# An even batch's leftover tokens held for the odd batch's tile, and the first batch's convolution and value products in other slots

## The chip, the cores and the metric

The kernel runs on one NeuronCore of one Trainium2 chip. The metric is device time in microseconds, the median over executions of the whole program. Before the change it is 1050.89 us, median of 3 runs (1049.84 to 1052.85). All arithmetic is in fp32; products marked fp32r use a high and a low part of each operand.

## What is computed

For 4 batches of 576 tokens, three blocks run one behind the other. The first is attention with 8 heads of 64 that keeps only the 32 largest scores of each row; the second a gated block with a causal convolution over tokens; the third a Fourier mixing with a normalisation and a two-layer network:

```python
scores = scale * np.matmul(q, k.transpose(0, 1, 3, 2))
kth = np.partition(scores, -top_k, axis=-1)[..., -top_k:-top_k + 1]      # top_k = 32
attn = softmax(np.where(scores >= kth, scores, -1e9));  x = attn @ v     # x: (4, 576, 512)

gate_pre += conv_w[k] * xp[:, k:k + S, :]                                # 5 taps
x = (1 / (1 + exp(-gate_pre)) * (x @ w_val)) @ w_out

mixed = np.real(np.fft.fft(np.fft.fft(x, axis=1), axis=2))
u = x + mixed
un = (u - mean(u)) / sqrt(var(u) + 1e-6)
out = u + np.maximum(un @ w_ch1, 0) @ w_ch2                              # 512 -> 2048 -> 512
```

## The kernel before

**Slots.** The whole program is one list of slots, and each engine walks through it in its own instruction stream. Slot s starts the scores of attention tile s. There are 16 pairs of heads with 9 tiles each, so 36 tiles a batch and 144 in all. The stages of one tile lie behind each other by slots: VectorE's search for the 32 largest (`search`, L1007: four MAX8 and three MATCH_REPLACE8 per tile) one and two slots later, the exponential on ScalarE four later, the transposes of the probabilities on TensorE five later (L588), and the product with v (`attend`, L591) six later.

**The two later blocks of a batch** are a list of steps (`STEPS`, L109), spread by `steps_by_slot` (L160) over the 36 slots that follow a batch's attention, so batch 0's steps lie in slots 42 to 77, beside batch 1's attention. Each step has an estimated cost (`COST`, L117), and the planner fills the slots evenly by it. The steps are: `val` (8 value products), `zed` and `seq` (the Fourier mixing), `proj` (5 projections), `trn` (5 transposes of normalised tokens), `ch0` and `ch1` (the hidden layers over 16 chunks, for two groups of tiles). Batch 3 has no attention beside it; its steps have one slot each at the end.

**Row tiles.** 576 tokens are four tiles of 128 and 64 leftover tokens (`ROWS`, L47; `LEFT` is 64). Tile number 4 (`NR - 1`) is the leftover one. For an even batch its tokens lie in partitions 0 to 63, for an odd one in 64 to 127 (`half_of`, L74). Before the change both batches of a pair do `proj` 4, the normalisation and `trn` 4 on 64 tokens each, with results side by side in `un_hi`, `un_lo` and `u[4]`; the hidden layers over the leftover tokens are already run once for the pair, in the odd batch's `ch1` (`GROUPS`, L58).

**Around the projection.** `project` (L710) multiplies the gated values with w_out, 16 matmuls a tile. `sequence` (L693) makes the mixing sums, ScalarE copies them to `ab`, and GpSimd's `plus_minus` (L1225) makes `pm` of them. VectorE's `make_u` (L1071) adds both into `u[r]` and takes the statistics (bn_stats, bn_aggr), GpSimd's `deviation` (L1238) makes 1/sqrt of the variance, VectorE's `normalise` (L1088) writes `un`, TensorE transposes it (`transpose_un`, L729), ScalarE stores it twice (L923, L924) and GpSimd subtracts (L1257).

**First batch.** Its convolution is on TensorE with diagonal matrices (`convolve`, L625, placed by `CONV0_AT`, L145), its tanh reads the result from PSUM (`TANH0_AT`). Two value products of batch 0 are begun early, at slot 39 (`VAL0_AT`, L156, `early_values`, L652): 6 products, each of two instructions. For batches 1 to 3 the convolution is on VectorE: one instruction for each tap of a range of tokens (`CONV_AT`, L150; `conv`, L1055). Only the last pair's is cut into two ranges, FRONT (tokens 0 to 383) and BACK (384 to 575).

**Order within a slot** on TensorE (L796 to L814): scores, transposes, the first step, `attend`, the convolution, early values, the other steps. At slot 42 alone (`CONV_LAST`) the convolution stands ahead of the first step. On VectorE (L1138 to L1154): half of the search, the first step, the other half, the convolution, the other steps. Each engine works in order, so an instruction that waits holds all behind it.

**Start.** SyncE's queue issues two loads of k for head 0 and four of q and k for head 1 (L517 to L519), ScalarE's queue two of q for head 0 (L937). The low parts of the first keys are made on VectorE, those of the first queries of head 0 on GpSimd (`low_queries`, L1158).

## Time and profile before

| | us |
|---|---|
| median of 3 runs | 1050.89 |
| lowest, highest | 1049.84, 1052.85 |
| the profiled execution | 1052.33 |
| its span, first to last instruction | 1050.6 |

The profile is of one execution. Its engines are TensorE (PE; PEld is its weight loads), VectorE (DVE), ScalarE (ACT), GpSimd (POOL) and SyncE (SP), whose stream only issues transfers. Busy time of PE is the union of instructions whose ends are modelled, so a PE that is nearly always busy need not be at its peak rate.

Attention's search ends near 857 us of the span; from there only batch 3's steps run. The steps of batch 0 start near 211 us, those of batch 1 near 427 us, of batch 2 near 666 us.

### The profile page before, as it was taken

The page shows a single profiled execution, that of the slowest core. Times are in us where ns is not written, and L with a number is a line of the kernel's source. Part 1 is how long each engine was busy: PE and PEld are TensorE (multiplying, and loading weights), DVE is VectorE, ACT ScalarE, POOL GpSimd, SP SyncE. Part 2 cuts the span into 40 slices and gives each one's busy share as a digit, 9 for nine tenths or more (in the row PEclk, how much of TensorE's full clock was granted, in tenths as well). Part 3 has the DMA queues.
Part 4 walks back from the last instruction along what each step waited for, and adds up shares of the span by engine and source line. Part 5 has one row for each costly group of instructions (what it writes and reads, how often), then busy time and mean ns, then how long its engine had stood idle before and what let it go on. Part 6 is the DMA issues. An engine that isn't in the chain of part 4 may idle for free.

```text
span 1050.6 us, 20124 instructions
## 1 busy us (share of the span) xinstructions
PE 972.2 (93%) x6784; PEld 831.6 (79%) x6784; DVE 839.0 (80%) x1824; ACT 647.2 (62%) x1421; POOL 408.2 (39%) x544
## 2 busy tenths in 40 slices
PE   4876767899999999999999999999999999999997
PEld 3555655678888898878898889878888888888896
DVE  7999999988999999989999977898999973120000
ACT  5887687856777767665777666666676762122121
POOL 2675544534533333244333332243442222543221
PEclk9997688799999999999999999999999999999999
DMA  9565656560186778511777655510676776059873
GB/s 237 181 202 167 220 185 200 173 215 24 26 293 228 284 265 293 177 35 34 274 269 259 200 202 198 163 35 24 214 262 244 261 252 231 1 199 358 297 248 129
DMA packets 84549, 203.80 MB, mean 194 GB/s; under 512 B 9056, under 2 KB 30304, under 8 KB 84448
## 3 DMA queue, kind: packets, MB, share of 16 engines
q1 hardware_dynamic: 84288, 202.22, 57.2%
q8 instruction: 55, 0.90, 0.4%
q10 hardware_dynamic: 160, 0.30, 0.1%
q14 instruction: 46, 0.38, 0.1%
HBM read 178.89 MB, written 23.59 MB: 193 GB/s over the span
## 4 chain that ended last, share of the span: by engine, by line
PE 77%; DVE 8%; issue 6%; ACT 6%; POOL 1%; DMA 0%; SPq 0%; ACTq 0%; DVEq 0%; POOLq 0%
PE p_m L757 18%; PE p_m L774 18%; PE p_t L604 9%; PE p_t L588 7%; PE p_s L574 7%; PE p_m L725 5%; PE p_m L647 4%; DVE rest L1004 3%; DVE top L993 3%; PE p_m L615 3%; PE p_m L706 3%; PE p_m L635 2%; PE p_t L608 2%; ACT prob L852 1%; ACT pT L866 1%
## 5 line engine op out<-in xcount | busy, mean ns | idle before, releaser
L993 DVE MAX8 top<-rest 128x8 f32<-128x576 f32 x432 | 310.3, 746 | 0.1
L1266 POOL TENSOR_TENSOR hid_lo<-hid,hid_hi 128x256 fp32r<-128x256 f32 (+1 forms) x128 | 107.5, 840 | 298.2 <-ACT hid_hi L934 298.2
L1004 DVE MATCH_REPLACE8 rest<-top,rest 128x576 f32<-128x576 f32 x288 | 214.1, 744 | 0.0
L774 PE MATMUL p_m<-w_st,hid_hi 128*128 128x512 f32 x576 | 181.3, 396 | 1.6 <-ACT hid_hi L934 0.7
L757 PE MATMUL p_m<-un_hi,w_st 128*128 128x256 f32 (+1 forms) x1024 | 164.2, 303 | 0.0
L840 ACT ACTIVATE s_sb<-p_s 128x576 f32<-128x576 f32 x144 | 93.1, 647 | 105.5 <-PE p_s L574 105.3
L757 PEld LDWEIGHTS p_m<-un_hi,w_st 128*128 128x128 f32 x1024 | 143.5, 188 | 5.6 <-issue 1.9
L588 PE MATMUL p_t<-id_sb,prob 128*128 128x128 f32 x720 | 111.6, 288 | 27.6 <-ACT prob L858 27.2
L933 ACT ACTIVATE hid<-p_m 128x256 f32<-128x256 f32 (+1 forms) x128 | 51.8, 405 | 128.5 <-PE p_m L757 127.6
L604 PE MATMUL p_t<-pT,v_sb 128*64 128x128 f32 (+1 forms) x1600 | 108.6, 288 | 22.9 <-ACT pT L866 22.9
L604 PEld LDWEIGHTS p_t<-pT,v_sb 128*64 128x64 f32 x1600 | 89.0, 149 | 48.6 <-ACT pT L866 29.6
L574 PE MATMUL p_s<-k_hi,q_st 128*128 128x288 f32 x320 | 108.9, 355 | 14.9 <-POOL q_st L1164 8.8
L858 ACT ACTIVATE prob<-prob,bias 128x576 f32<-128x576 f32 x144 | 111.8, 776 | 16.8 <-ACT prob L852 0.8
L588 PEld LDWEIGHTS p_t<-id_sb,prob 128*128 128x128 f32 x720 | 90.1, 148 | 35.4 <-ACT prob L858 33.9
L774 PEld LDWEIGHTS p_m<-w_st,hid_hi 128*128 128x128 f32 x576 | 101.1, 188 | 18.6 <-POOL hid_lo L1266 2.9
L774 PE MATMUL p_m<-w_st,hid_lo 128*128 128x512 f32 x288 | 113.6, 394 | 0.0
L993 DVE MAX8 top<-s_sb 128x8 f32<-128x576 f32 x144 | 108.8, 755 | 3.7 <-ACT s_sb L840 3.6
L852 ACT ACTIVATE prob<-s_sb,top 128x576 f32<-128x576 f32 x144 | 110.9, 770 | 0.0
L1004 DVE MATCH_REPLACE8 rest<-top,s_sb 128x576 f32<-128x576 f32 x144 | 107.1, 744 | 0.0
L866 ACT ACTIVATE pT<-p_t 128x640 f32<-128x640 f32 x144 | 101.3, 704 | 8.6 <-PE p_t L588 8.4
L1100 DVE TENSOR_TENSOR u<-p_m,u 128x512 f32<-128x512 f32 x18 | 11.5, 684 | 111.3 <-PE p_m L774 111.3
L574 PE MATMUL p_s<-k_lo,q_st 128*128 128x288 f32 x320 | 94.5, 310 | 0.0
(117 smaller groups left out, 1650.3 us busy)
## 6 DMA issues: line engine op xcount, KB each, us to landing
w_st<-w_split SPq DMA_DIRECT2D x256, 512.0 KB, 4.6
w_split<-w_st SPq DMA_DIRECT2D x32, 512.0 KB, 3.3
k_raw<-kT SPq DMA_DIRECT2D x62, 144.0 KB, 3.0
q_raw<-qT SPq DMA_DIRECT2D x60, 144.0 KB, 2.9
u<-w_ch SPq DMA_DIRECT2D x32, 256.0 KB, 3.9
v_sb<-v SPq DMA_DIRECT2D x16, 256.0 KB, 3.1
w_st<-wout_split SPq DMA_DIRECT2D x16, 256.0 KB, 3.9
out<-u SPq DMA_DIRECT2D x16, 256.0 KB, 2.4
```

The lines of the kernel that those rows point to most:

```text
L574: mm = pe.matmul(p_s[:, o, 0:HALF_S], q_st[h][p % 2][:, cols], k[:, o * HALF_S:o * HALF_S + HALF_S], start=n == 0, stop=n == len(parts) - 1)
L588: mm = pe.transpose(p_t[:, c * P:c * P + P], prob[t % 3][:, c * P:c * P + P], id_sb[:, :])
L604: pe.matmul(p_o[D * h:D * h + D, 0, 0:n], v_sb[p % 2][:, c, D * h:D * h + D], pT[tt % 3][:, c, c0:c0 + n], start=c == 0, stop=c == NCH - 1 ...
L757: mm = pe.matmul(mbank(hidden_bank(b, g, f), n), w1_st[i % NB1][:, w, k, :], x[:, k, at:at + n], start=part + k == 0, stop=part + k == KC + 1)
L774: mm = pe.matmul(mbank(j), h[i % 2][:, P * j:P * j + P], w2_st[i % NB2][:, w, :], start=f == 0 and part == 0, stop=f == FC - 1 and part == 2)
L840: act.activation(s_sb[t % NS][:, :].rearrange("p (o n) -> p o n", o=2), p_s[:, :, 0:HALF_S], ACT.Copy, scale=SCALE).then_inc(s_copy, 1)
L852: act.activation(prob[t % 3][:, 0:S], s_sb[t % NS][:, :], ACT.Prelu, bias=kth, scale=-1.0, alpha=1.0 / BIG).then_inc(s_drop, 1)
L858: act.activation(prob[t % 3][:, 0:S], prob[t % 3][:, 0:S], ACT.Exp, bias=bias[t % NK][:, :], scale=-BIG, accum_out=psum_row[:, t % NK:t % ...
L866: act.activation(pT[t % 3][:, :, :].rearrange("p c n -> p (c n)"), p_t[:, 0:SP], ACT.Copy).then_inc(s_pT, 1)
L993: found = dve.max(top[t % NK][:, 8 * n:8 * n + 8], (rest[t % 2] if n else s_sb[t % NS])[:, :])
L1004: chained(dve.match_replace(rest[t % 2][:, :], top[t % NK][:, 8 * n:8 * n + 8], (rest[t % 2] if n else s_sb[t % NS])[:, :], LOWEST), t)
L1266: pool.tensor_tensor(hid_lo[i % 2][:, 0:width(b, g)], hid[:, 0:width(b, g)], hid_hi[i % 2][:, 0:width(b, g)].bitcast(F32), ALU.subtract).t ...
```

## The change

An even batch leaves out `proj` 4 and `trn` 4. Its gated leftover values wait in `gv_hi` and `gv_lo`, its mixing sums for these tokens are written by GpSimd straight into `u[4]`, partitions 0 to 63. The odd batch's `proj` 4 then works on 128 tokens, one VectorE instruction adds the even half, and statistics, normalisation, transposes and the stores behind them run once on 128 tokens. The semaphore counts follow (`us`, `outs`). The planner spreads an even batch's remaining 56 steps anew.

Several other things are in the same change. The hidden layer of an even batch alternates between two PSUM banks from chunk 10 on, instead of 12 (`TRANSPOSED`). For batch 0 the convolution of the last pair's first half goes from slot 41 to 39, the second half stays at slot 42 but stands behind the first step, and the early value products go from slot 39 to slots 35 and 37, three products at each. The last tanh of batch 0 stands later in ScalarE's slot. For batches 1 to 3 the last pair's convolution is cut into three ranges: FRONT (384 tokens) at slots 39 and 40, NEXT (128) at 41 and BACK (64) at 42, instead of FRONT at 39 to 41 and BACK (192) at 42 (slots counted from the batch's start). At the start ScalarE's queue issues head 1's two loads of k, and VectorE makes the first low queries instead of GpSimd.

```diff
-CONV0_AT = {14: (0, 0), 16: (0, 1), 23: (1, 0), 25: (1, 1), 32: (2, 0), 34: (2, 1), 41: (3, 0), 42: (3, 1)}
-CONV_LAST = max(CONV0_AT)
+CONV0_AT = {14: (0, 0), 16: (0, 1), 23: (1, 0), 25: (1, 1), 32: (2, 0), 34: (2, 1), 39: (3, 0), 42: (3, 1)}
-WHOLE, FRONT, BACK = (0, S), (0, 3 * P), (3 * P, S)
+WHOLE, FRONT, NEXT, BACK = (0, S), (0, 3 * P), (3 * P, 4 * P), (4 * P, S)
-           39: [(3, FRONT, (0, 1))], 40: [(3, FRONT, (2, 3))], 41: [(3, FRONT, (4,))], 42: [(3, BACK, range(TAPS))]}
-CONVS = TAPS * (KC + 1)
-VAL0_AT, VAL0 = 39, 2
+           39: [(3, FRONT, (0, 1, 2))], 40: [(3, FRONT, (3, 4))], 41: [(3, NEXT, range(TAPS))], 42: [(3, BACK, range(TAPS))]}
+CONVS = TAPS * (KC + 2)
+VAL0_AT = {35: 0, 37: 1}
...
+LAST_TILE = [("proj", NR - 1), ("trn", NR - 1)]
-        steps = [(what, b, n) for what, n in STEPS]
+        steps = [(what, b, n) for what, n in STEPS if b % 2 or (what, n) not in LAST_TILE]
...
+TRANSPOSED = [10, 12]
-        return 3 if f == 1 or f >= 12 and f % 2 == 0 else 2
+        return 3 if f == 1 or f >= TRANSPOSED[b % 2] and f % 2 == 0 else 2
...
-                load_qk(0, 1)
+                for half in range(2):
+                    sp.dma_start(raw(0, 1)[0][D * half:D * half + D, :], qT[0, 1]).then_inc(s_qk_in[1], 16)
...
-                    bank = mbank(PROJ_BANK[r])[out_rows(b, r), :]
+                    bank = mbank(PROJ_BANK[r])
...
-                    if s == CONV_LAST:
-                        convolve(*CONV0_AT[s])
                     for x in plan[s][0:1]:
                         step(*x)
                     if unit_due(s):
                         attend(s - ATTEND)
-                    if s in CONV0_AT and s != CONV_LAST:
+                    if s in CONV0_AT:
                         convolve(*CONV0_AT[s])
-                    if s == VAL0_AT:
-                        early_values()
+                    if s in VAL0_AT:
+                        early_values(VAL0_AT[s])
...
+                for half in range(2):
+                    act.dma_start(raw(0, 1)[1][D * half:D * half + D, :], kT[0, 1]).then_inc(s_qk_in[1], 16)
                 high_keys(0, 0)
...
-                    if s in TANH0_AT:
+                    if TANH0_AT.get(s, KC - 1) < KC - 1:
                         gate_tanh(0, TANH0_AT[s])
...
+                    if TANH0_AT.get(s) == KC - 1:
+                        gate_tanh(0, KC - 1)
...
+                    at, made = slice(0, P), us(b) + 2 * (r + 1)
+                    if r == NR - 1:
+                        at, made = rows(b, r), us(b + 1)
+                        early = rows(b - 1, r)
+                        dve.tensor_tensor(u[r][early, :], y[early, :], u[r][early, :], ALU.add).then_inc(m_u, 1)
+                    ur = u[r][at, :]
                     dve.tensor_tensor(ur[:, 0:NCOS], y[at, 0:NCOS], pm[at, lo, :], ALU.add).then_inc(m_u, 1)
                     dve.tensor_tensor(ur[:, NCOS:DM], y[at, NCOS:DM], pm[at, hi, NCOS - 2:0:-1], ALU.add).then_inc(m_u, 1)
-                    dve.wait_ge(m_u, 2 * (NR * b + r + 1))
-                    dve.bn_stats(stats[at, r, :], ur).then_inc(m_st, 1)
+                    dve.wait_ge(m_u, made)
+                    dve.bn_stats(stats[:, r, :], u[r][:, :]).then_inc(m_st, 1)
...
+                dve.wait_ge(s_hi, 2)
+                dve.tensor_tensor(q_st[0][0][0:D, 0:S], q_raw[0:D, :], q_st[0][0][0:D, 0:S].bitcast(F32),
                                   ALU.subtract).then_inc(s_lo[0], 1)
                 low_queries(0)
...
+                    a, bb = ab[at, 1:NCOS - 1], ab[at, NCOS:DM]
+                    if g == 2 and b % 2 == 0:
+                        if b:
+                            pool.wait_ge(m_put, 16 * puts(b))
+                        to = u[NR - 1][at, :]
+                        pool.tensor_tensor(to[:, 1:NCOS - 1], a, bb, ALU.subtract).then_inc(m_pm, 1)
+                        pool.tensor_tensor(to[:, DM - 1:NCOS - 1:-1], a, bb, ALU.add).then_inc(m_pm, 1)
+                        for n in (0, NCOS - 1):
+                            pool.tensor_copy(to[:, n:n + 1], ab[at, n:n + 1]).then_inc(m_pm, 1)
+                        return
...
                 pool.wait_ge(s_zero, FILLS)
-                low_queries(0, 0)
```

## Rows read from the trace of the kernel before

**Rows 1.** The page, part 1: busy us, share of the span, instructions.
```profile
PE 972.2 (93%) x6784; PEld 831.6 (79%) x6784; DVE 839.0 (80%) x1824; ACT 647.2 (62%) x1421; POOL 408.2 (39%) x544
```

**Rows 2.** Windows: stretch, its us, each engine's busy us, PE clock, DMA share, GB/s.
```profile
0.00:198.00 198.00, 139.90 (x874) 109.38 (x875) 190.32 (x409) 147.44 (x301) 101.45 (x133) 0.83 0.64 197
198.00:208.80 10.80, 9.20 (x85) 7.58 (x84) 9.79 (x21) 9.62 (x22) 7.68 (x10) 0.98 0.47 165
208.80:272.00 63.20, 62.10 (x421) 51.94 (x420) 54.70 (x129) 39.82 (x86) 25.37 (x38) 1.00 0.31 106
272.00:453.00 181.00, 176.35 (x1395) 153.56 (x1393) 179.73 (x390) 128.03 (x292) 65.40 (x85) 1.00 0.67 232
453.00:473.00 20.00, 19.86 (x116) 17.14 (x117) 15.56 (x35) 14.45 (x30) 11.03 (x14) 0.91 0.00 1
497.00:608.00 111.00, 109.97 (x849) 98.40 (x849) 107.17 (x224) 77.56 (x177) 41.59 (x52) 1.00 0.73 246
664.00:693.00 29.00, 27.04 (x195) 21.79 (x191) 28.79 (x69) 17.96 (x39) 8.30 (x12) 1.00 0.40 122
728.00:861.00 133.00, 130.75 (x1048) 114.89 (x1047) 130.06 (x279) 96.49 (x222) 44.63 (x61) 1.00 0.68 232
```

**Rows 3.** The chain that ended last, start: start us, length us, what.
```profile
4.18 4.23 DMA x_new<-kT
```

**Rows 4.** The page, part 6: issues, KB each, median us to landing.
```profile
k_raw<-kT SPq DMA_DIRECT2D x62, 144.0 KB, 3.0
```

**Rows 5.** Timeline at the start: start, us, engine, line, operation, [idle before, releaser].
```profile
8.54 0.61 PE L574 MATMUL p_s<-k_hi,q_st 128*128 128x288 f32 x1 [8.54 <-POOL q_st L1164]
9.98 0.74 DVE L1038 TENSOR_TENSOR k_lo<-x_new,k_hi 128x576 fp32r<-128x576 f32 x1
```

**Rows 6.** Timeline, slots 39 to 43.
```profile
198.28 3.15 PE L647 MATMUL p_m<-x_new,wslot 128*128 128x257 f32 x12
...
207.89 2.69 PE L635 MATMUL p_m<-x_new,u 128*128 128x288 f32 x10
...
208.85 0.17 DVE L1051 TENSOR_SCALAR rinv<-psum_row 128x2 f32<-128x2 f32 x1 [0.98 <-ACT prob L858]
...
211.49 2.59 PE L635 MATMUL p_m<-x_new,u 128*128 128x288 f32 x10
...
214.56 0.42 DVE L1113 SCALAR_TENSOR_TENSOR gv<-gate,p_m 128x257 f32<-128x257 f32 x1 [2.56 <-PE p_m L647]
...
216.66 0.77 PE L588 MATMUL p_t<-id_sb,prob 128*128 128x128 f32 x5 [1.07 <-ACT prob L858]
```

**Rows 7.** The chain that ended last, batch 0's projection of tile 4.
```profile
280.58 2.80 PE p_m L725 x16
```

**Rows 8.** Timeline: tile 4 of batch 0 on DVE; a 64-token transpose on PE.
```profile
285.93 0.41 DVE L1081 TENSOR_TENSOR u<-p_m,pm 64x257 f32<-64x257 f32 x1
...
287.52 1.38 DVE L993 MAX8 top<-rest 128x8 f32<-128x576 f32 x2
...
321.94 0.53 DVE L1094 TENSOR_SCALAR un<-u,mv,rstd 64x512 f32<-64x512 f32 x1
322.39 1.41 DVE L993 MAX8 top<-rest 128x8 f32<-128x576 f32 x2
...
957.15 0.46 PE L742 MATMUL p_m<-id_sb,un 64*128 64x64 f32 x4
```

**Rows 9.** Groups by line and shape: operation, shape, count, busy us, mean ns, idle.
```profile
L1067 DVE SCALAR_TENSOR_TENSOR gate<-x_new,cw_sb,gate 128x384 f32<-128x384 f32 x12 | 9.2, 766 | 0.2
...
L1067 DVE SCALAR_TENSOR_TENSOR gate<-x_new,cw_sb,gate 128x192 f32<-128x192 f32 x12 | 5.0, 419 | 0.4
...
L1113 DVE SCALAR_TENSOR_TENSOR gv<-gate,p_m 128x63 f32<-128x63 f32 x16 | 3.4, 213 | 6.0 <-PE p_m L647 6.0
```

**Rows 10.** Timeline at the start of batch 1's and batch 2's steps.
```profile
453.14 0.65 PE L682 MATMUL p_m<-wfeat,gv 128*64 128x257 f32 x4 [2.57 <-DVE gv L1113]
...
693.40 1.12 PE L682 MATMUL p_m<-wfeat,gv 128*64 128x257 f32 x4 [2.36 <-DVE gv L1113]
```

More of the change, by code:

```diff
@@ L394, in folded, with tile_cols @@
             return gate[:, c, o * HALF + P * m:o * HALF + P * m + P]
[L396 to L401 removed]
+        def tile_cols(r):
+            return slice(ROWS[r][0], ROWS[r][0] + P)
         def w_out_half(b, k, h):
@@ L650, in value_products, with early_values @@
                     return mm
-                def early_values():
+                def early_values(j):
                     pe.wait_ge(m_wval, 16)
                     pe.wait_ge(s_feat_ev, KC)
-                    for j in range(VAL0):
-                        value_products(0, j, range(KC - 1))
+                    value_products(0, j, range(KC - 1))
                 def values(b, j):
@@ L672, in values @@
                         pe.wait_ge(m_tanh, KC)
-                    value_products(b, j, range(KC - 1 if b == 0 and j < VAL0 else 0, KC)).then_inc(m_val, 1)
+                    value_products(b, j, range(KC - 1 if b == 0 and j in VAL0_AT.values() else 0, KC)).then_inc(m_val, 1)
                 def zed(b, m):
@@ L724, in project @@
                             for c0, c1, w in w_out_half(b, k, h):
-                                mm = pe.matmul(bank[:, c0:c1], x[:, k, gv_cols(b, r)], w, start=n + k == 0,
+                                mm = pe.matmul(bank[:, c0:c1], x[:, k, tile_cols(r)], w, start=n + k == 0,
                                                stop=n == 2 and k == KC - 1, skip_group_check=True)
@@ L751, in hidden @@
                         pe.wait_ge(m_hev, hidden_before(i) + 1)
-                    if g == 0 and f == 12:
-                        pe.wait_ge(m_unT, 2 * NR * (b + 1))
+                    if g == 0 and f == TRANSPOSED[b % 2]:
+                        pe.wait_ge(m_unT, 2 * outs(b + 1))
                     at, n = HALF * g, width(b, g)
@@ L1057, in conv @@
                     n0, n1 = part
-                    dve.wait_ge(s_x, 5 * p + (3 if part == FRONT else 5))
+                    dve.wait_ge(s_x, 5 * p + {FRONT: 3, NEXT: 4}.get(part, 5))
                     if c == 0:
@@ L1072, in make_u @@
                     g = [0, 0, 1, 1, 2][r]
-                    at = rows(b, r)
                     lo, hi = (1, 0) if r in (1, 3) else (0, 1)
@@ L1117, in step @@
                         finish(b, int(what == "ch1"))
-                    if (what, n) in NORM_AT:
+                    if (what, n) in NORM_AT and outs(b) + NORM_AT[what, n] < outs(b + 1):
                         normalise(b, NORM_AT[what, n])
```

79 lines of the change are left out of this document (35 added, 44 removed).

## The prediction

> **What bounds the kernel now.** The first view is the busy shares of the page. TensorE reads 93% and VectorE 80% [rows 1], and taken over the whole span this would make the case one of TensorE's work alone. It does not hold stage by stage, so the second view is the busy time by windows [rows 2]. The reader is to look there for the engine whose busy time equals the length of the stretch.
>
> Up to 198 us it is VectorE. The table shows 190.3 of 198 us busy, and the missing part is the start, before the first scores. TensorE has 139.9 and its clock is granted at 0.83 of full, a mixture of 1.2 and 2.4 GHz. From 208.8 to 272 us it is TensorE: 62.1 of 63.2, while VectorE stands idle for 8.5 us. From 272 to 453 us both columns are nearly full, and here the two have to be told apart: VectorE lacks 1.3 us of 181, TensorE 4.7 us. So VectorE sets the end of that stretch and TensorE follows with some slack. The same holds from 728 to 861 us (VectorE lacks 2.9, most of it at the very end where its search is over, TensorE 2.3) and from 664 to 693 us (0.2 against 2.0). In 497 to 608 us neither has more than 4 us.
>
> The Trainium skill, Perfetto Trace Analysis, section Identifying the Most-Contended Engine, says that busy matmul time is no good measure for TensorE and that the busy share of weight loads should be read instead, with plain occupancy for VectorE. In this case's trace that is 79% against VectorE's 80% [rows 1], which goes with two engines that take turns. By the other reading, TensorE everywhere, the sum would be that of the first rival below.
>
> The third view is the timeline at the places where one engine waits for the other, used below.
>
> **The start.** ScalarE's queue takes over two of head 1's four loads. Today the last of the four is issued at 4.18 us and lands 4.23 us later [rows 3], against a median of 3.0 us for such loads [rows 4], so it stands in line behind the others and an earlier issue shortens little. The four issues on SyncE are 0.64 us apart, so two fewer ahead of the last one can give at most 1.3 us, and at worst nothing. I take 0.2, near the row that shows the line. VectorE also takes over the low queries that TensorE's first scores wait for [rows 5]. It costs one operation of about 0.75 us, and there VectorE is idle and waits for head 1's data. Its last operation before the search begins, at 9.98 us [rows 5], depends on that data and not on the first scores. Cover gone, it would cost 0.75 us. **Sum: 0.2 gained.**
>
> The Trainium skill, Trainium Kernel Development and Optimization, section Key Constraints, says that queues of several engines interleave on the same 16 DMA engines and save only the issue time. By it the gain is at most the 1.3 us of issue. The row of 4.23 us says less.
>
> **Slots 35 to 43, batch 0.** Today slot 39 holds 12 instructions of early value products, 3.15 us [rows 6]. In their place comes half a convolution, 10 instructions, 2.69 us [rows 6]. So slot 39 does not get longer as long as the clock is the same. The value products go to slots 35 and 37, where TensorE waits for the exponentials: it is idle for 58 of the 198 us before [rows 2], which is 1.5 us a slot over 39 slots. Half of them last 1.6 us at full clock, about 3 at half. What these two slots can't hide is some tenths, and the scores that follow have slack because VectorE is behind. I cost them at nothing; with no cover it would be 3 us.
>
> Slot 41 loses its convolution, 2.69 us, so scores 42 come that much earlier. In slot 42 the other half, 2.59 us, no longer stands ahead of the first value product, for which VectorE waits 2.56 us today [rows 6]. TensorE's wait of 1.07 us for an exponential [rows 6] goes too, because ScalarE's last tanh, which waits for the convolution, now stands behind that exponential. From slot 43 on TensorE is the bound, so it counts: 2.69 and 1.07 are 3.8 at most. VectorE's idle time up to there, 0.98 and 2.56 [rows 6], is 3.5, and it can't come further forward than that without becoming the late one. **I take 3.3, with 0.5 and 3.8 as ends.** What is late next is TensorE's own list of value products.
>
> **The leftover tile in an even batch.** On TensorE there go 16 matmuls, 2.80 us [rows 7], and 4 transposes, 0.46 [rows 8], together 3.3 us. On VectorE the tile occupies 285.93 to 287.52, which is 1.59 us, and its normalisation 321.94 to 322.39, 0.45 us [rows 8]: together 2.04 us. Both lie in a stretch where VectorE is the late engine, so 2.04 counts and TensorE's other 1.3 us become idle time. ScalarE and GpSimd lose work too; their busy shares of 62 and 39% [rows 1] leave that without effect. **Twice 2.0 is 4.1 us gained**, with 3.3 each as the upper end.
>
> In the odd batch nothing is saved. VectorE has one more addition, over 512 columns; by the 257-column one of 0.41 us [rows 8] it takes some 0.7. In batch 1 it lies ahead of the stretch from 497 us, where VectorE has under 4 us of room [rows 2], so between 0 and 0.7, and I take the middle: **0.35 lost**. In batch 3 it lies beside GpSimd's work and costs nothing. The transposes take 128 columns for 64, and weight loads as well: **0.15 lost** in the tail, where TensorE is alone. GpSimd's `plus_minus` in an even batch has as many instructions as before. For batch 2 it waits for the stores of batch 1, issued some ten slots earlier; behind it in GpSimd's stream stand low parts of the next keys, and nobody waits for them at once. SyncE's two waits for the last projection come one projection sooner, and the weight loads and query loads behind them too. The bank alternation from chunk 10 takes away waits on TensorE in a stretch where it has slack: nothing.
>
> **Narrow convolution, batches 1 to 3.** On VectorE five taps of 192 columns (0.42 us each [rows 9], 2.1 together) become five of 128 and five of 64. A 63-column instruction of the same kind takes 0.21 [rows 9] and between the two I get 0.33 for 128, so the ten take 2.7 us: 0.6 more. The ends are 0.3, by the slope from 384 to 192 columns (766 to 419 ns), and 2.1, if a narrow one costs as much as one of 192. In batch 1 it stands in VectorE's stretch: **0.6 lost**. For batch 2 the extra lies ahead of 664 us, where TensorE is the bound, and what remains behind is five taps of 64 for five of 192, 1.0 us less. There TensorE waits 2.36 us for the gated values [rows 10]: **1.0 gained**. For batch 3 it falls to the end of the search and is hidden.
>
> **Sum:** 0.2 + 3.3 + 4.1 - 0.35 - 0.15 - 0.6 + 1.0 = 7.5 us. Of the profiled execution, 1052.33 us with a span of 1050.6, this leaves 1044.8; the median of the runs is 1.4 us below that execution, so I predict 1043.4 us.
>
> **Rivals.**
>
> First, TensorE sets the pace everywhere. For it speaks its 93%, and that removed waits of VectorE may let it run without gaps. Against it speaks VectorE's 179.7 of 181 us. Then each even batch gives 3.3, and VectorE's added work costs nothing: 0.2 + 3.3 + 6.6 - 0.15 + 1.0 = 11.0, or 1039.9 us. A further 1.8 us comes if the clock no longer falls behind the wait at 453.14 [rows 10]: the stretch from 453 to 473 us has 0.91 for a clock [rows 2], that is 3.6 us at 1.2 GHz and 1.8 lost.
>
> Second, the opening gives little. Today the clock is 0.98 from 198 us on [rows 2], right behind a dense slot. With the value products spread over slots 35 and 37 it may still be at 1.2 GHz at slot 39, and the convolution then lasts 5.4 us for 2.7. That takes the 3.3 down to 0.5: 4.7 in all, or 1046.2 us. The Trainium skill, TensorE: Matmul & The Clock Gate, section Part 1, says that the throttled clock is the default and activity releases it; this speaks against taking work out of slot 39, and would give this time if nothing replaced it. The convolution does replace it there, 10 instructions for 12.
>
> Third, the change doesn't do what it says: the narrow taps cost like wide ones (2.1 more in each batch at its most loaded slots) and the saved tile of an even batch turns into waiting at the start of the next batch, where TensorE already waits 2.57 us for VectorE [rows 10]. 7.5 - 1.5 - 1.0 - 2.0 is 3.0 or less, 1047.9 to 1051 us.
>
> Fourth, slower: TensorE's slack in batches 1 and 2's attention grows from 4.7 to some 6 us, and its clock falls there. Two falls stand in the dense part today, each behind a wait of over 2.3 us [rows 10], and none behind the wait of 1.07 us [rows 6]. Each costs 1.8 us by the sum above as long as TensorE then becomes the late engine. It decides from four new falls on, which use up the gain, and with six it is 3.3 us slower, 1054.2 us. Against it, TensorE lacks only 4.7 us in the whole of 272 to 453 us.
>
> **How the numbers follow.** My forecast has 0.50, TensorE everywhere 0.17, little from the opening 0.13, no effect 0.13, slower 0.07. The forecast's own bounds (0.5 to 3.8 for the opening, 0 to 1.3 for the start, 0.3 to 2.1 for the taps) reach from 1041.5 to 1047. The range 1038.5 to 1048.5 takes in the first two rivals and the edge of the third, and leaves out the fourth, most of the third and a small part of the first. About 0.3%, 3.15 us, can be told from no change. Faster by more than that: forecast, first and second, 0.80. Within it: 0.13. Slower: 0.07.
>
> **What would show it.** In the trace of the changed kernel the steps of batch 1 should start some 3.5 + 2 - 0.6, about 5 us earlier than at 427 us; those of batch 0 should start near 209 us, with VectorE's wait of 2.56 gone and no convolution right ahead of slot 42's scores. VectorE should stay without idle time in what is now 272 to 453 us, with TensorE's idle time risen to 5 or 6 us. If instead TensorE's stays under 5 and the stretch shrinks by over 3 us, the first rival is right. If the convolution at slot 39 shows about 5 us, the second is. The 64-column taps should show 0.2 to 0.25 us each. At the start of batch 2's steps TensorE's wait should be near 1.4 instead of 2.36. The prediction is wrong if the clock falls in more places than two, or if the shift of the first 211 us is not there.

## The result, and the profile after

| | before | after |
|---|---|---|
| median of 18 runs each, same chip | 1049.86 | 1053.29 |
| lowest, highest | 1046.02, 1052.85 | 1050.26, 1055.05 |
| ratio, 95% interval | 1 | 1.0035 [1.0023, 1.0046] |
| the profiled execution, its span | 1052.33, 1050.6 | 1052.68, 1050.9 |

The change makes the kernel 3.7 us slower, where 7.5 us of gain were forecast. The time, 1053.29 us, lies above the range of 1038.5 to 1048.5.

The page of after, its head and part 1, against [rows 1]:

```profile
span 1050.9 us, 20032 instructions
PE 964.3 (92%) x6744; PEld 825.4 (79%) x6744; DVE 839.1 (80%) x1832; ACT 644.7 (61%) x1417; POOL 404.5 (38%) x537
```

TensorE has less to do and the span did not shrink. So the next view is a comparison by stage. A turnover is here the place where one batch's steps end and the next batch's begin. A mark that both kernels have is the first MAX8 of a tile's search. Here and below, stretch A runs from that of tile 48 to that of tile 81 (batch 0's steps from its mixing on), stretch B from that of tile 123 to that of tile 143 (most of batch 2's). Windows of both in before, columns as in [rows 2]:

```profile
252.51:455.85 203.34, 198.55 (x1556) 172.92 (x1555) 198.67 (x434) 141.20 (x321) 76.14 (x107) 1.00 0.61 210
735.37:849.10 113.73, 111.83 (x898) 98.97 (x897) 113.03 (x245) 81.35 (x188) 38.98 (x54) 1.00 0.71 241
```

and in after:

```profile
244.99:453.17 208.18, 197.89 (x1530) 172.43 (x1529) 198.25 (x433) 139.61 (x317) 74.02 (x104) 0.98 0.60 205
730.95:849.08 118.13, 111.47 (x878) 99.19 (x877) 111.30 (x240) 80.83 (x188) 38.97 (x53) 0.97 0.66 231
```

The reader should take length less busy time, which is an engine's idle time. Tile 48 is searched 7.5 us earlier than before (244.99 for 252.51), so the opening delivered, though the last section shows that half of this difference is the clock of this one trace. Then stretch A is 4.8 us longer and stretch B 4.4 us longer, and in each VectorE, which had 4.7 and 0.7 us of idle time, now has 9.9 and 6.8. At tile 143 the lead is 0.0. (Between the stretches it had grown by 1.7 us, 1.3 of it at the turnover near 693 us, where the clock falls in before and not in after.) Both stretches are those of an even batch, where the leftover tile was taken out. Where in them? The timeline of after at the end of batch 0's projections (slots 52 to 54):

```profile
270.55 1.56 POOL L1179 TENSOR_TENSOR q_st<-q_raw,q_st 64x512 fp32r<-64x512 f32 x2
272.08 1.26 POOL L1281 TENSOR_TENSOR un_lo<-un,un_hi 128x512 fp32r<-128x512 f32 x1
273.72 1.25 POOL L1281 TENSOR_TENSOR un_lo<-un,un_hi 128x512 fp32r<-128x512 f32 x1
275.03 1.21 PE L763 MATMUL p_m<-un_hi,w_st 128*128 128x256 f32 x8 [2.19 <-POOL un_lo L1281]
276.78 0.38 ACT L936 ACTIVATE hid<-p_m 128x256 f32<-128x256 f32 x1 [3.20 <-PE p_m L763]
...
278.40 0.78 ACT L862 ACTIVATE prob<-prob,bias 128x576 f32<-128x576 f32 x1
279.32 1.33 PE L597 MATMUL p_t<-id_sb,prob 128*128 128x128 f32 x5 [1.61 <-ACT prob L862]
```

Two waits of TensorE follow each other. The first hidden chunk waits 2.19 us for GpSimd's second `un_lo`, the low parts of the second normalised tile. ScalarE then waits 3.20 us to store that chunk and does the exponential only behind it, so the next transposes wait 1.61 us more. Batch 2 has the same pair (2.21 and 1.67). Windows of after behind the first wait, in batch 0 and in batch 2:

```profile
276.50:283.40 6.90, 5.29 (x24) 4.88 (x24) 6.90 (x17) 3.70 (x9) 2.18 (x3) 0.51 0.53 134
737.30:744.20 6.90, 5.23 (x25) 4.88 (x25) 6.90 (x16) 3.61 (x8) 2.80 (x5) 0.51 0.42 118
```

Behind the first wait the granted clock is 0.51, the lower level, for 6.9 us in both batches. Here is the same place in before, where TensorE does not wait:

```profile
277.01 1.55 POOL L1164 TENSOR_TENSOR q_st<-q_raw,q_st 64x512 fp32r<-64x512 f32 x2
278.52 1.28 POOL L1257 TENSOR_TENSOR un_lo<-un,un_hi 128x512 fp32r<-128x512 f32 x1
280.19 1.29 POOL L1257 TENSOR_TENSOR un_lo<-un,un_hi 128x512 fp32r<-128x512 f32 x1
280.34 0.48 PE L725 MATMUL p_m<-w_out,un_hi 128*64 128x512 f32 x1
282.29 0.78 ACT L858 ACTIVATE prob<-prob,bias 128x576 f32<-128x576 f32 x1
283.22 1.11 PE L757 MATMUL p_m<-un_hi,w_st 128*128 128x256 f32 x8
284.84 0.38 ACT L933 ACTIVATE hid<-p_m 128x256 f32<-128x256 f32 x1 [1.68 <-PE p_m L757]
```

The second `un_lo` ends at 281.48. TensorE does projection 4 from 280.34 until chunk 0 starts at 283.22, and the exponential ends at 283.1, while the projection still runs. **The removed projection was the cover of both.** Two side effects of the edit make it worse. The planner, with two steps fewer, puts projection 2 one slot later (51 for 50), so its normalisation and low parts come later. And chunk 0 now is the first step of slot 53. ScalarE stores a slot's first step ahead of the exponential if it is a chunk.

Theory: this lost cover (with the order on the two helpers and the clock behind it) takes away what the rest of the change gives. Rivals: the opening or the narrow taps lose (the prediction's second and third), or the merge itself gives nothing because the other engine sets the pace.

### The profile page after: what moved, and what is told of

It is laid out like the page before. It is cut to its first block, busy times and chain, and to the rows that moved or that the text cites. A ratio compares the mean times of both kernels' runs of the same rounds, so it can differ in the third digit from the quotient of the medians.

```text
span 1050.9 us, 20032 instructions
## 1 busy us (share of the span) xinstructions
PE 964.3 (92%) x6744; PEld 825.4 (79%) x6744; DVE 839.1 (80%) x1832; ACT 644.7 (61%) x1417; POOL 404.5 (38%) x537
## 4 chain that ended last, share of the span: by engine, by line
PE 55%; DVE 28%; issue 11%; POOL 3%; ACT 2%; DMA 1%; SPq 0%; DVEq 0%; ACTq 0%; POOLq 0%
PE p_m L763 17%; PE p_m L780 16%; DVE rest L1012 13%; DVE top L1001 11%; PE p_t L613 4%; PE p_t L597 4%; PE p_s L583 3%; PE p_m L733 3%; PE p_m L624 3%; PE p_m L714 2%; PE p_m L656 1%; POOL hid_lo L1289 1%; DVE gv L1125 1%; PE p_t L617 1%; DVE gate L1075 1%
## 5 line engine op out<-in xcount | busy, mean ns | idle before, releaser
L763 PE MATMUL p_m<-un_hi,w_st 128*128 128x256 f32 (+1 forms) x1024 | 166.6, 305 | 4.4 <-POOL un_lo L1281 4.4
L597 PE MATMUL p_t<-id_sb,prob 128*128 128x128 f32 x720 | 109.4, 284 | 24.9 <-ACT prob L862 24.9
L613 PE MATMUL p_t<-pT,v_sb 128*64 128x128 f32 (+1 forms) x1600 | 105.6, 282 | 24.9 <-ACT pT L870 24.9
L613 PEld LDWEIGHTS p_t<-pT,v_sb 128*64 128x64 f32 x1600 | 86.6, 146 | 49.4 <-ACT pT L870 31.1
```

The lines of the kernel that those rows point to most:

```text
L597: mm = pe.transpose(p_t[:, c * P:c * P + P], prob[t % 3][:, c * P:c * P + P], id_sb[:, :])
L613: pe.matmul(p_o[D * h:D * h + D, 0, 0:n], v_sb[p % 2][:, c, D * h:D * h + D], pT[tt % 3][:, c, c0:c0 + n], start=c == 0, stop=c == NCH - 1 ...
L763: mm = pe.matmul(mbank(hidden_bank(b, g, f), n), w1_st[i % NB1][:, w, k, :], x[:, k, at:at + n], start=part + k == 0, stop=part + k == KC + 1)
```

## The experiments

All ratios are to before, in runs on the same chip. Medians of before in the three sets were 1047.67, 1049.69 and 1049.45 us. A ratio's interval reaches 1.5 to 2.4 us to either side, so a difference of under some 3 us between two experiments rests on the traces and not on the times.

### First set: the parts of the change

**e_open**: before with the opening, the start and the narrow taps; the leftover tile as before.

```diff
+CONV0_AT = {..., 39: (3, 0), 42: (3, 1)}
+VAL0_AT = {35: 0, 37: 1}
+WHOLE, FRONT, NEXT, BACK = (0, S), (0, 3 * P), (3 * P, 4 * P), (4 * P, S)
```

> The kernel before with the opening, the start and the narrow convolution changed and the leftover tile as it was (both batches of a pair project and normalise it themselves, old plan of steps). Two theories. Cover theory: the trace of the changed kernel is 7.5 us ahead at slot 48 and 9.0 at slot 54, and only what follows is lost to the leftover edit, so this kernel keeps its lead to the end: 1041 to 1044 us. Rival (the lead is only lent): VectorE and TensorE are both full from slot 54 on, so whatever the opening wins is given back there anyway: 1047 to 1050 us.

Measured: 1047.40 us, ratio 0.9982 [0.9965, 0.9998]. That is the time that the rival had named (1047 to 1050), and not 1041 to 1044. The trace does not show the rival's mechanism, though. Its lead is the same at tile 51 and tile 69 (6.0 us), and 5.0 at tile 78, so it is not given back in the dense slots, and these parts lose 1.1 us late in stretch A. The forecast of 1041 to 1044 took the whole lead of 7.5 us for the change's own, which it is not (last section).

**e_left**: before with the leftover edit alone, with the planner's new slots.

```diff
+LAST_TILE = [("proj", NR - 1), ("trn", NR - 1)]
-        steps = [(what, b, n) for what, n in STEPS]
+        steps = [(what, b, n) for what, n in STEPS if b % 2 or (what, n) not in LAST_TILE]
```

> The kernel before with the leftover edit alone (one projection, normalisation and transposes for a pair, banks from chunk 10, the new plan of an even batch's steps), opening, start and convolution as they were. Cover theory: an even batch loses what slots 54 to 81 and 126 to 143 lose in the changed kernel, 6.3 and 4.7 us, so about 1059 us (1055 to 1062), with a wait of TensorE of 2 us or more for GpSimd's un_lo ahead of the first hidden chunk. Rival (lead only lent): 1048 to 1051 us, no net loss of its own.

Measured: 1056.72 us, ratio 1.0072 [1.005, 1.0095]. The loss sits in this part, as the first theory had it (1055 to 1062). It has the waits of 2.21 us (GpSimd) and 1.61 us (exponential) at chunk 0, and the clock falls there in both even batches.

**e_plan**: the changed kernel with the old slots. The two steps are planned as before and struck out afterwards.

```diff
+    for s in out:
+        out[s] = [x for x in out[s] if x[1] % 2 or (x[0], x[2]) not in LAST_TILE]
```

> The changed kernel with the slots of the steps as in the kernel before: the planner counts projection 4 and transposes 4 of an even batch, and they are struck out afterwards; nothing else differs. It tells the missing cover from the moved steps. If the new plan does the harm (projection 2 a slot later, two chunks in slots that had one): 1039 to 1043 us, TensorE's wait ahead of the first chunk under 1 us. If it is the missing 2.8 us of TensorE work over GpSimd's un_lo: the wait stays at about 2 us, the clock falls behind it, 1049 to 1053 us.

Measured: 1047.74 us, ratio 0.9997 [0.9979, 1.0016], 0.0038 under that of after. It lies between the two theories, 1039 to 1043 and 1049 to 1053, so slots and cover both have a part. The wait for GpSimd falls from 2.19 to 0.95 us, the wait for the exponential rises to 2.04:

```profile
275.48 1.21 PE L765 MATMUL p_m<-un_hi,w_st 128*128 128x256 f32 x8 [0.95 <-POOL un_lo L1283]
279.75 0.77 PE L599 MATMUL p_t<-id_sb,prob 128*128 128x128 f32 x5 [2.04 <-ACT prob L864]
```

**e_cover**: the same, but TensorE does 16 matmuls into an unused bank in place of the even batch's projection 4. This is added work whose result nobody reads; VectorE, ScalarE and GpSimd stay without the tile. The edit changes a second thing. The useless projection is again the first step of slots 53 and 125, so chunk 0 no longer is, and ScalarE does the exponential ahead of it as in before.

```diff
+                    elif what == "proj" and n == NR - 1 and b % 2 == 0:
+                        cover(b)
```

> As the one before (old slots), and TensorE again does 16 matmuls of the old projection's shape in an even batch at the old place, into a bank nobody reads: the cover without its result. If cover or plan do the harm, the wait for un_lo is gone, the clock does not fall there and the time is 1038 to 1042 us: the opening's 8 us and up to 2 us of VectorE's saved work. If the harm lies elsewhere in the leftover edit (128-token statistics, GpSimd writing u, the odd batch), it stays at 1049 to 1053 us. Against the kernel before it: if the cover was free TensorE time, both show the same time or this one is faster; if it costs its 2.8 us twice, this one is 5.6 us slower.

Measured: 1046.64 us, ratio 0.998 [0.9962, 0.9999]. Forecast were 1038 to 1042. 2.8 us of useless work in each even batch make it no slower than e_plan, rather faster (0.0017, inside the intervals). Both waits and the clock fall behind them are gone:

```profile
245.45:449.22 203.77, 197.63 (x1546) 171.77 (x1545) 198.87 (x433) 139.80 (x317) 73.94 (x103) 0.99 0.61 209
729.73:843.13 113.40, 110.94 (x894) 98.65 (x893) 112.56 (x240) 81.03 (x186) 37.43 (x51) 1.00 0.71 242
```

VectorE's idle time is back at 4.9 and 0.8. So the absence of the tile on the other engines is not the cause. What the run can't tell apart are the cover and ScalarE's order, since it brings back both. The next set does that.

### Second set: the two orders mended, at the old slots

**e_act**: e_plan, and ScalarE does not store an even batch's chunk 0 ahead of the exponential.

```diff
-first = any(what == "ch0" and n < 12 for what, b, n in plan[s][0:1])
+first = any(what == "ch0" and (n or b % 2) and n < 12 for what, b, n in plan[s][0:1])
```

> The kernel e_plan (changed kernel, old slots) with one edit in ScalarE's order: in slots 53 and 125 the first hidden chunk of an even batch no longer stands ahead of the exponential. Without projection 4 that chunk became the first step of its slot, and ScalarE stores a first step ahead of the exponential; in e_plan TensorE then waits 2.0 us for the exponential at 279.75 us, after 0.95 us for GpSimd. Order theory: the 2.0 us and the fall of the clock behind it (1.7 us) go in each even batch, 7 us in all, so 1040 to 1043 us. Rival: the exponential was late anyway, because the chain through TensorE and GpSimd is the long one: 1046 to 1048 us, the wait only moves to ScalarE's chunk.

Measured: 1046.10 us, ratio 0.9967 [0.9948, 0.9985]. The wait for the exponential is gone, the one for GpSimd (0.92) stays, and the clock does not fall there. VectorE's idle time is 4.7 and 0.8, as in before. The gain over e_plan is 0.0030, 3.1 us, and not the 7 us of the order theory; the time lies in the rival's range (1046 to 1048), but its sign, a wait that only moves, is not there.

**e_pool**: e_plan, and GpSimd makes the next head's low queries of slots 51 and 123 one slot later, behind the projection's low parts.

```diff
+                    if s - 1 in HELD:
+                        low_queries(*split_at(s - 1, LOW_Q0, LOW_Q))
```

> The kernel e_plan with one edit in GpSimd's order: the low queries of slots 51 and 123 (1.55 us) come behind the steps of the next slot, so the two un_lo of 1.3 us that the first hidden chunk waits for start some 1.4 us sooner. TensorE's wait of 0.95 us for un_lo should vanish. GpSimd theory (this wait starts the trouble): 1043 to 1045 us. Order theory (ScalarE's order is the main part): the chunk is stored up to 1 us sooner and so is the exponential behind it, 2 us gained in all, 1045 to 1047 us, with a wait of 1.1 us or more left at the exponential.

Measured: 1047.05 us, ratio 0.998 [0.9962, 0.9997]. The wait for GpSimd is gone, the one for the exponential stays (2.04 and 2.10), and behind it the clock falls in batch 2. VectorE's idle time is 4.7 and 0.8 here too. So with the old slots either wait by itself leaves VectorE without added idle time, and only both together (e_plan, 9.3 and 2.8) don't. TensorE's slack covers one of them. (Stretch B of e_pool is 1.2 us longer than that of e_act all the same, in VectorE's busy time: with the low queries moved, a small instruction of VectorE waits for GpSimd's next one and lasts 1.63 us. The next section comes to such instructions.)

**e_both**: both edits. 

> Both edits together, in old slots. If TensorE sets the pace and the removed 2.8 us of projection were lost only to these two waits, each even batch gives 2.8 to 3.3 us over the kernel e_cover, which has neither wait but does the work: 1039 to 1041 us against its 1046.6. If VectorE sets the pace from slot 54 on, as my prediction had it, no more than 0 to 1 us under e_cover: 1045 to 1047 us, with VectorE free of idle time.

Measured: 1045.95 us, ratio 0.9967 [0.995, 0.9985]. The timeline shows all three engines in the new order:

```profile
270.89 1.27 POOL L1284 TENSOR_TENSOR un_lo<-un,un_hi 128x512 fp32r<-128x512 f32 x1
272.53 1.29 POOL L1284 TENSOR_TENSOR un_lo<-un,un_hi 128x512 fp32r<-128x512 f32 x1
274.19 1.19 PE L766 MATMUL p_m<-un_hi,w_st 128*128 128x256 f32 x8
276.13 0.78 ACT L865 ACTIVATE prob<-prob,bias 128x576 f32<-128x576 f32 x1
276.91 0.36 ACT L939 ACTIVATE hid<-p_m 128x256 f32<-128x256 f32 x1
277.05 0.77 PE L600 MATMUL p_t<-id_sb,prob 128*128 128x128 f32 x5 [0.67 <-ACT prob L865]
```

The second `un_lo` ends ahead of chunk 0, and the exponential stands ahead of the chunk's store. One wait of 0.67 us is left, for e_plan's 0.95 and 2.04. Against e_plan the two edits give 0.0030 (3.1 us; the two intervals overlap by 0.0006). By the times e_act alone does as well as both; the intervals can't tell the two apart. The time is what was forecast if VectorE sets the pace (1045 to 1047). If TensorE did, it would be 1039 to 1041.

**b_again**: before once more, one execution. 

> The kernel before once more, for a second trace. Its executions lie between 1045 and 1053 us, and the trace that the prediction was read from is one of 1052.3. If the opening's lead of 7.5 us at slot 48 was read against an unusually slow opening, this trace is ahead of the first one by slot 48 whenever it is a shorter one. If not, its opening is the same within 1 us and the difference arises later.

Measured: 1045.52 us, span 1043.7. Stretches A and B have the lengths of before (203.34 and 113.83 against 203.34 and 113.73), but tile 48 is searched at 248.67 and not at 252.51. The last section comes back to this.

### Third set: slots, taps and the merge alone

**e_bothnew**: e_both with the planner's new slots. 

> The changed kernel with its own list of slots (the second projection one slot later, chunk 0 first in its slot) and both order edits: ScalarE doesn't store an even batch's chunk 0 ahead of the exponential, and GpSimd makes the keys' and queries' low parts of the slots before chunk 0 only after the projection's. Nothing is left out of the computation. Theory one, the loss is in the order of the two helpers: as the kernel with the old slots and both edits, a ratio to before of 0.996 to 0.998, no wait of TensorE over 1.2 us between 262 and 300 us, the clock at full there. Theory two, the new slots themselves cost: the second projection comes a slot later, so TensorE still waits about 1 us for the low parts that GpSimd makes of its norm; ratio 0.999 to 1.001, and a clock fall of 3.4 us or more behind that wait.

Measured: 1050.30 us, ratio 1.0013 [0.9996, 1.003].

```profile
246.98:451.99 205.01, 196.32 (x1534) 171.03 (x1532) 198.27 (x433) 139.92 (x319) 73.79 (x104) 1.00 0.61 208
729.86:845.25 115.39, 109.47 (x878) 97.11 (x877) 110.98 (x239) 80.71 (x188) 39.35 (x53) 1.00 0.69 236
```

The second theory nearly holds in size (it had 0.999 to 1.001), though not in its way: against e_both the new slots cost 0.0046 (4.8 us) and no clock fall goes with it. TensorE waits 0.69 us for GpSimd, and VectorE's idle time is 6.7 and 4.4. The largest piece of it stands at the end of a later slot of batch 0's chunks:

```profile
326.77 0.39 ACT L937 ACTIVATE hid<-p_m 128x256 f32<-128x256 f32 x1 [0.79 <-PE p_m L764]
328.39 0.78 ACT L863 ACTIVATE prob<-prob,bias 128x576 f32<-128x576 f32 x1
329.29 0.17 DVE L1060 TENSOR_SCALAR rinv<-psum_row 128x2 f32<-128x2 f32 x1 [1.65 <-ACT prob L863]
```

Here it is a later chunk that ScalarE stores ahead of the exponential, and VectorE waits for the sum. e_both, with the old slots, has no such wait of VectorE. No run changed the order at this place, so that the new slots cost is shown, and how they do it is read from this trace alone.

**e_wide**: e_both with the wide taps of before. 

> The kernel with the old slots and both order edits, but with the wide convolution of before on VectorE (five taps of 192 columns in the last part). Nothing is left out of the computation. Theory one, the narrow taps lose about 1.1 us at the most loaded slots of batch 1, because ten instructions take longer than five: this kernel keeps its lead between the 69th and the 78th tile of the search, and is 0.5 to 1.5 us faster than the one with narrow taps, about 1045 us. Theory two, the 0.6 us that the forecast gave for batch 1 is given back with 1.0 at batch 2's turnover: then this kernel is 0.4 us slower, and TensorE waits longer at the start of batch 2's steps than with narrow taps.

Measured: 1043.04 us, ratio 0.995 [0.9934, 0.9966], the fastest of all, 5 us faster than before. The first theory is right in kind: tiles 69 to 78 keep their lead (6.6 and 6.5 us against the first trace of before, where e_both falls from 7.1 to 6.1). In size it was low: 1.8 us by the ratios, 2.9 by the medians. The intervals of the two kernels overlap, so the size is uncertain.

```profile
246.72:448.81 202.09, 195.17 (x1528) 169.82 (x1527) 197.60 (x428) 139.59 (x316) 73.73 (x103) 0.99 0.61 211
727.06:839.97 112.91, 109.04 (x878) 96.74 (x877) 112.08 (x240) 80.95 (x186) 37.24 (x51) 1.00 0.69 243
```

**e_leftm**: before with the merge alone, old slots, both orders mended, wide taps. 

> The kernel before with the merge of the leftover tiles alone, in the old slots and with both order edits: opening, start and convolution are those of before. Nothing is left out of the computation. Against the same merge with the new slots and no order edit, which gave a ratio of 1.0072. Theory one, the removed projection gives TensorE's own 3.3 us in each even batch once its cover is replaced: 6 us in all, ratio 0.994 to 0.996. Theory two, VectorE's 2.04 us: 4 us in all, ratio 0.996 to 0.997. Theory three, part of the gain turns into the waits of 0.4 to 0.9 us that are left at chunk 0, and a dense stretch gives the rest back at the turnovers: 1 to 3 us, ratio 0.997 to 0.999.

Measured: 1047.00 us, ratio 0.998 [0.9964, 0.9997]. Of the three theories the third fits: 2.1 us for both batches.

```profile
250.61:453.56 202.95, 195.94 (x1536) 170.82 (x1535) 198.23 (x428) 140.81 (x319) 74.26 (x104) 1.00 0.61 210
732.90:845.89 112.99, 108.79 (x878) 96.63 (x876) 112.16 (x239) 81.02 (x186) 37.25 (x51) 1.00 0.69 243
```

**e_narrow**: before with the narrow taps alone. 

> The kernel before with the narrow convolution alone. Nothing is left out of the computation. The forecast's step: 0.6 us lost in batch 1, 1.0 gained at batch 2's turnover, together 0.4 faster, ratio 0.9996. Rival: 1.1 us lost in batch 1 and nothing gained at the turnover, where TensorE's wait stays at 2.4 us or more, ratio 1.001. Either is near the limit of what times can tell, so the trace decides: the start of the search of tiles 69 to 78 and TensorE's wait at the start of batch 2's steps.

Measured: 1051.01 us, ratio 1.0027 [1.0012, 1.0042]. The rival was right in sign and at the turnover; its 1.001 lies just under the interval. Its groups of VectorE by shape:

```profile
L1067 DVE SCALAR_TENSOR_TENSOR gate<-x_new,cw_sb,gate 128x128 f32<-128x128 f32 x12 | 4.2, 352 | 0.4
L1067 DVE SCALAR_TENSOR_TENSOR gate<-x_new,cw_sb,gate 128x64 f32<-128x64 f32 x12 | 3.4, 285 | 0.4
```

and its timeline at the start of batch 1's and batch 2's steps, where [rows 10] has 2.57 and 2.36:

```profile
450.42 1.13 PE L682 MATMUL p_m<-wfeat,gv 128*64 128x257 f32 x4 [2.91 <-DVE gv L1113]
691.15 0.66 PE L682 MATMUL p_m<-wfeat,gv 128*64 128x257 f32 x4 [2.97 <-DVE gv L1113]
```

All stretches side by side, worked out from each kernel's windows (idle is length less busy time of VectorE and TensorE):

| kernel | tile 48 | A | DVE, PE idle | B | DVE, PE idle |
|---|---|---|---|---|---|
| before | 252.51 | 203.34 | 4.7, 4.8 | 113.73 | 0.7, 1.9 |
| b_again | 248.67 | 203.34 | 4.7, 4.8 | 113.83 | 0.7, 2.1 |
| e_narrow | 248.79 | 203.82 | 4.9, 5.6 | 113.45 | 0.7, 1.9 |
| e_open | 246.78 | 204.10 | 4.6, 5.6 | 113.42 | 0.7, 1.9 |
| e_leftm | 250.61 | 202.95 | 4.7, 7.0 | 112.99 | 0.8, 4.2 |
| e_wide | 246.72 | 202.09 | 4.5, 6.9 | 112.91 | 0.8, 3.9 |
| e_cover | 245.45 | 203.77 | 4.9, 6.1 | 113.40 | 0.8, 2.5 |
| e_act | 244.67 | 203.34 | 4.7, 7.6 | 113.27 | 0.8, 4.4 |
| e_pool | 244.70 | 203.61 | 4.7, 8.2 | 114.49 | 0.8, 4.6 |
| e_both | 246.38 | 203.39 | 4.9, 7.2 | 111.84 | 0.8, 3.1 |
| e_bothnew | 246.98 | 205.01 | 6.7, 8.7 | 115.39 | 4.4, 5.9 |
| e_plan | 246.48 | 206.66 | 9.3, 9.1 | 114.39 | 2.8, 5.5 |
| e_left | 252.29 | 207.49 | 10.1, 9.5 | 117.81 | 6.6, 7.1 |
| after | 244.99 | 208.18 | 9.9, 10.3 | 118.13 | 6.8, 6.7 |

Each row is one trace. A time of tile 48 holds the clock of that trace's opening, so it differs by up to 3.8 us between executions of one kernel (before and b_again), while A and B agree to 0.1 us.

## Why the prediction was wrong, point by point

**The pace of stretches A and B: right.** Wherever the waits are mended, VectorE's idle time is what it was (4.5 to 4.9 and 0.8) while TensorE's rises, by 2.0 to 2.3 us a stretch in e_leftm and e_wide. TensorE has room there, VectorE has not. The first rival, TensorE everywhere, is refuted: e_leftm takes its 3.3 us away in each even batch, and 2.2 and 2.3 us of it show up as TensorE's idle time; e_both, 1045.95 us, says the same.

**The leftover tile: the step that failed.** The prediction took 3.3 us from TensorE and 2.04 from VectorE and called the rest without effect. It did not ask what the 2.80 us of projection 4 [rows 7] covered. They covered the low parts of the second tile on GpSimd and the exponential on ScalarE, and with them gone TensorE waits 2.2 and 1.6 us. Part of this is not the missing time itself but the order: chunk 0 became the first step of its slot, and ScalarE's store of it went ahead of the exponential. e_act changes that order alone, without any cover, and VectorE's added idle time is gone. The prediction did not carry the list of steps through the planner either, which moved projection 2 and the chunks. Measured, these are two terms that the sum has not: the order of the two helpers 0.0030 (e_plan to e_both, 3.1 us) and the new slots 0.0038 to 0.0046 (e_plan to after, e_both to e_bothnew, 4.0 to 4.8 us). Both together, from e_both to after, are 0.0068, 7.1 us lost.

**Its size was off too.** With everything mended the merge gives 2.1 us [0.3, 3.8] (e_leftm) and not 4.1. In stretches A and B it is 0.4 and 0.7 us. Part of the missing rest is visible in VectorE's recorded busy time, which falls by 0.4 us in stretch A where 2.04 us of work are gone. In e_wide, the same merge, a small instruction shows where it went:

```profile
297.53 1.62 POOL L1182 TENSOR_TENSOR q_st<-q_raw,q_st 64x576 fp32r<-64x576 f32 x1
297.78 1.40 DVE L1062 TENSOR_SCALAR rinv<-psum_row 128x2 f32<-128x2 f32 x1
```

`rinv`, two columns, lasts 1.40 us where the row of e_bothnew above has 0.17, and it ends at 299.18, GpSimd's instruction at 299.15. In e_leftm it lasts 1.39 at both even batches. So VectorE stood behind GpSimd. The Trainium skill, SBUF — State Buffer, section SBUF: two separate sides, says that the two engines share a pair of ports under an exclusive lock, for some of VectorE's operations, and that the other one is blocked for the whole instruction; the rows agree to 0.03 us. A lengthened instruction counts as busy, so this loss doesn't show in VectorE's idle time.

One trace shows the stretch without it. In batch 2 of e_both no `rinv` lasts longer than 0.28 us, in e_act one lasts 0.70 and one 0.94, each ending with an instruction of GpSimd. Stretch B of e_both and of e_act:

```profile
728.38:840.22 111.84, 108.70 (x878) 96.62 (x877) 111.00 (x240) 81.04 (x186) 37.49 (x51) 1.00 0.69 246
729.69:842.96 113.27, 108.87 (x878) 96.70 (x877) 112.44 (x240) 81.08 (x186) 37.29 (x51) 1.00 0.68 242
```

Against before (113.73, VectorE 113.03 busy) e_both's stretch B is 1.9 us shorter and VectorE's busy time 2.03 us less, which is the 2.04 that was forecast for a batch. In e_leftm that stretch is 0.7 us shorter, 1.3 short of the forecast, and the one `rinv` is 1.2 us too long. So VectorE's 2.04 us of work were counted rightly, and a wait of this kind takes most of them away. No experiment moved one such instruction by itself, so the shares are argued, not shown.

**The opening: right in size and mechanism.** Forecast 3.3 and 0.2 for the start. e_leftm and e_wide differ in the opening and the start alone: 1047.00 and 1043.04, which is 4.0 us by the medians and 3.1 by the ratios. The second way is the search of tile 48: it starts at 250.6 in the mean of the five traces with the old opening and at 245.9 in that of the nine with the new, 4.7 us. The two halves of the convolution in after, of slots 39 and 42, and the first gated values:

```profile
193.19 2.69 PE L644 MATMUL p_m<-x_new,u 128*128 128x288 f32 x10 [0.21 <-POOL x_new L1208]
204.50 2.59 PE L644 MATMUL p_m<-x_new,u 128*128 128x288 f32 x10
209.74 0.41 DVE L1125 SCALAR_TENSOR_TENSOR gv<-gate,p_m 128x257 f32<-128x257 f32 x1
```

The half at slot 39 lasts 2.69 us, and 2.59 to 2.69 in all nine traces with the new opening, not 5.4. So the second rival is refuted. The gated values begin at 209.74 for 214.56, and VectorE's wait of 2.56 us [rows 6] is gone. That wait was partly the clock of the one trace that was read: in b_again it is 0.93, and the gated values begin at 210.72. After is ahead of b_again by 1.0 us at tile 42 (212.57 for 213.56) and by 3.7 at tile 48.

**The start: nothing.** Forecast 0.2. The last load is issued at 2.89 us for 4.18, and takes longer:

```profile
2.89 5.56 DMA x_new<-qT
```

It lands at 8.45, before at 8.41 [rows 3]. The first search starts 0.05 us later than before.

**Narrow taps: wrong sign.** Forecast 0.6 lost in batch 1 and 1.0 gained at batch 2's start, 0.4 gained. Measured 1.6 us lost by the medians of e_narrow, 2.8 by the ratio, 1.8 from e_both to e_wide; the traces of before and e_narrow, counted from tile 69 on, give 1.4 (the clock falls at both turnovers in both; b_again, without a fall, is no match). Two things failed. A tap of 64 columns costs 285 ns and one of 128 costs 352. The forecast had 213 and 330, from the 63-column instruction in [rows 9], which is the same operation on other operands. So ten taps cost 1.1 us more than five and not 0.6. And at batch 2 the extra was said to lie ahead of the stretch that counts. It does not. TensorE's wait there rises to 2.96 to 2.98 in every kernel with narrow taps and is 2.35 or 2.36 in every kernel with wide ones, against the 1.4 forecast. The row that would have warned is in [rows 2]: VectorE had 0.2 us idle in 664 to 693. The forecast's bounds had a slip as well: with 0.5 for the opening, nothing for the start and 2.1 for the taps the gain is 3.0 us, which is 1047.9 and not 1047.

**The fourth rival** named the sign and half the mechanism: waits that make the clock fall. Its condition, four new falls, was not met. Two suffice, because each comes with some 3.8 us of waiting, which the rival counted at nothing. e_plan gives the price of a fall by itself. Its even batches have the same two waits (0.95 and 2.04, 0.96 and 2.10), and the clock falls in batch 0 only. There VectorE's idle time rises by 4.6, in batch 2 by 2.1 us, so the fall costs 2.5 us there, where 1.8 was forecast. That is no fixed price. In e_pool's batch 2 the clock falls behind one wait of 2.10 us and VectorE's idle time stays at 0.8. The prediction's own sign for being wrong, clock falls in more than two places, did show: after has them near 276.5, 450.6 and 737.3 us.

**Bank alternation and SyncE's earlier loads** were costed at nothing. No experiment undid them alone. In e_leftm TensorE waits once in each stretch for a load of weights (0.95 and 1.07 us), and VectorE's idle time doesn't rise with it.

The terms by the ratios, along one chain of kernels: merge 2.1 gained (before to e_leftm), opening 3.1 gained (to e_wide), taps 1.8 lost (to e_both), order 3.1 lost (to e_plan), slots 4.0 lost (to after). The chain ends at 3.7 us slower by construction, so the total checks nothing, and each term is uncertain by some 2 us.

## What to carry to other kernels

Work that is removed from one engine is also time in which others finished something. Before it is counted as a gain, list for the step behind it what it waits for and when that ends: here the second `un_lo` ended at 281.48 and projection 4 at 283.2, so 1.1 us of the 2.8 was already spoken for on GpSimd alone. An experiment that puts the removed work back needs the same question: what else comes back with it, as here the order on ScalarE. If a planner places the steps, run its list for the new kernel and compare slots, since a step that moves one slot can cost more than the step that went. And if an edit changes which step is first in a slot, look at every engine that treats the first one in its own way.

## What the runs showed of the hardware

The times of the unchanged kernel lie between 1045 and 1053 us, and the two traces of it show where the difference arises. The search of tiles 0 to 33 starts at the same times to 0.05 us. Then windows of before over the opening and the two turnovers:

```profile
195.00:210.00 15.00, 13.40 (x108) 11.16 (x105) 13.91 (x31) 12.02 (x28) 9.34 (x12) 0.89 0.47 165
450.00:460.00 10.00, 7.43 (x36) 5.84 (x32) 9.96 (x23) 4.63 (x10) 4.78 (x7) 0.83 0.16 42
690.00:700.00 10.00, 7.64 (x39) 5.82 (x35) 9.96 (x24) 8.14 (x17) 3.39 (x4) 0.83 0.02 7
```

and of b_again:

```profile
195.00:210.00 15.00, 13.40 (x106) 10.98 (x105) 14.75 (x33) 10.83 (x24) 6.84 (x9) 1.00 0.46 164
450.00:460.00 10.00, 10.00 (x66) 8.89 (x68) 9.97 (x22) 9.77 (x21) 5.62 (x7) 1.00 0.00 0
690.00:700.00 10.00, 10.00 (x68) 8.67 (x67) 9.96 (x23) 6.68 (x14) 4.63 (x6) 1.00 0.00 0
```

The waits at the turnovers are equal in both executions (2.57 and 2.36), yet the clock falls behind them in one and not in the other. Tile 48 is 3.8 us later in before; the turnover at 453 costs it 1.7 us more and the one at 693 another 1.3, together 6.8 us, the difference of the two spans. A lead read from one pair of traces may thus be half chance, by how the clock fell in each: of the 7.5 us that after leads by at tile 48, b_again leaves 3.7.
